# Causal convolution and token-mixing MLP on one core: x in 128-token chunks, convolution in 64x64 tiles, a VectorE block transpose, gated stores

## The reference, cut to what matters

```python
w = softmax(weight)                                   # 8 heads x 7 taps
y[b, s, h, g] = sum_k w[h, k] * x_pad[b, s + k, h, g] # 6 zeros ahead of each batch
W_tok = 1/8 * (y @ w_q) @ (y @ w_k).T                 # 4224 x 4224, a batch
out = relu(W_tok @ y) @ w_out                         # 4224 x 192, f32
```

## Time and profile before

| what | us |
|---|---|
| three runs | 170.98, 170.24, 170.30 |
| the profiled execution: its span, first to last instruction | 168.6 |
| median of the runs less that span: what lies around it | 1.7 |
| TensorE matmul busy | 158.3 (94% of the span) |
| TensorE weight loads busy (beside the matmuls) | 116.1 |
| ScalarE busy | 123.8 (73%) |
| VectorE busy | 116.2 (69%) |
| GpSimd busy | 30.3 |
| HBM read, written | 27.56 MB, 25.95 MB |

### The profile page before, as it was taken

How to read it: one execution, slowest core, us unless ns; L and a number is a source line. 1 busy time by engine, 2 the same in 40 slices (tenths; PEclk the granted TensorE clock), 3 DMA queues, 4 the chain that set the end, 5 groups by cost and what they waited for, 6 DMA issues and landing times.

```text
span 168.6 us, 6398 instructions
## 1 busy us (share of the span) xinstructions
PE 158.3 (94%) x2874; PEld 116.1 (69%) x2882; DVE 116.2 (69%) x201; ACT 123.8 (73%) x207; POOL 30.3 (18%) x39
## 2 busy tenths in 40 slices
PE   6978999999999999999999999999999999999980
PEld 1458846876677886777865867787778777884640
DVE  5745878774678777566999686875957758578640
ACT  3233699798977869888566978578897889568970
POOL 7999553530503120000000000000000000000000
PEclk9999999999999999999999999999999999999997
DMA  2999999999999999999999999996644463095897
GB/s 23 172 190 185 205 191 196 189 241 301 263 328 208 300 268 276 299 251 317 284 287 199 289 282 341 235 273 232 231 176 190 189 257 149 0 368 218 315 363 283
DMA packets 48154, 40.31 MB, mean 239 GB/s; under 512 B 37632, under 2 KB 40960, under 8 KB 48128
## 3 DMA queue, kind: packets, MB, share of 16 engines
q0 software_dynamic: 36128, 13.61, 67.6%
q1 hardware_dynamic: 12000, 26.31, 43.1%
HBM read 27.56 MB, written 25.95 MB: 317 GB/s over the span
## 4 chain that ended last, share of the span: by engine, by line
PE 78%; ACT 8%; DMA 4%; DVE 3%; issue 2%; POOL 1%; POOLq 0%; ACTq 0%
PE ps L744 14%; PE ps L902 12%; PE ps L920 9%; PE ps L316 8%; PE ps L321 5%; PE ps L836 5%; DMA out_dram<-out_sb 4%; PE ps L678 4%; PE ps L707 4%; ACT y L621 4%; PE ps L711 3%; PE ps L856 3%; PE ps L315 3%; PE ps L322 3%; PE ps L317 2%
## 5 line engine op out<-in xcount | busy, mean ns | idle before, releaser
L621 ACT CAST y<-ps 122x864 bf16<-122x864 f32 (+3 forms) x48 | 37.2, 794 | 11.6 <-PE ps L315 5.8
L873 ACT ACTIVATE rt<-ps 128x1024 bf16<-128x1024 f32 (+3 forms) x56 | 38.7, 725 | 8.3 <-PE ps L836 6.8
L941 ACT COPY out_sb<-ps 128x768 f32<-128x768 f32 (+1 forms) x43 | 32.6, 779 | 11.9 <-PE ps L920 11.3
L513 POOL DMA_DIRECT2D xw<-in_x_dram x34 | 29.9, 909 | 29.4 <-issue 28.6
L941 DVE COPY out_sb<-ps 128x768 f32<-128x768 f32 (+1 forms) x29 | 23.9, 831 | 14.0 <-PE ps L920 12.7
L744 PEld LDWEIGHTS ps<-y 122*64 122x64 bf16 x840 | 29.4, 110 | 5.3 <-issue 2.2
L744 PE MATMUL ps<-y 122*64 122x64 bf16 (+3 forms) x840 | 32.8, 221 | 0.1
L648 DVE COPY ytl<-ps 128x976 bf16<-128x976 bf16 (+1 forms) x40 | 23.3, 592 | 7.2 <-PE ps L321 4.1
L621 DVE CAST y<-ps 122x816 bf16<-122x816 f32 (+3 forms) x24 | 21.5, 902 | 8.1 <-PE ps L317 5.4
L316 PE MATMUL ps<-xw,band 128*64 128x408 bf16 (+2 forms) x104 | 24.9, 342 | 0.0
L317 PE MATMUL ps<-xw,band 128*64 128x408 bf16 (+2 forms) x104 | 24.9, 342 | 0.0
(11 more groups left out here) (117 smaller groups left out, 209.8 us busy)
## 6 DMA issues: line engine op xcount, KB each, us to landing
out_dram<-out_sb SPq DMA_DIRECT2D x28, 768.0 KB, 7.3
xw<-in_x_dram POOLq DMA_DIRECT2D x7, 816.0 KB, 40.3
xw<-in_x_dram POOLq DMA_DIRECT2D x7, 768.0 KB, 42.9
out_dram<-out_sb SPq DMA_DIRECT2D x8, 384.0 KB, 3.1
xw<-in_x_dram POOLq DMA_DIRECT2D x2, 432.0 KB, 7.3
out_dram<-out_sb SPq DMA_DIRECT2D x8, 96.0 KB, 5.1
xw<-in_x_dram POOLq DMA_DIRECT2D x1, 384.0 KB, 5.1
xw<-in_x_dram POOLq DMA_DIRECT2D x8, 45.8 KB, 28.0
```

The source lines that it names most:

```text
L513: lambda e, op, part=part: e.dma_start(*part),
L621: return e.copy(dst, src) if op.engine == "ACT" else e.tensor_copy(dst, src)
L873: return e.activation(dst, src(), AF.Relu)
L941: return e.copy(dst, src) if op.engine == "ACT" else e.tensor_copy(dst, src)
```

## The change

The whole program is declared and ordered anew; the arithmetic is the same.

- **Load.** A batch is 33 chunks of 128 tokens, each row read once, in 4 pieces (9, 8, 8, 8 chunks). `XW` is a ring of 3 batches with one zero chunk ahead, and a load waits until the convolution of three batches earlier has read its part.
- **Convolution.** 64x64 tiles: a chunk's lower and upper 64 rows are two row tiles, the 64 new outputs of each half two column tiles. A pair of heads takes two phases of four matmuls, one in each quadrant; the second (`conv_2`) adds into what the first wrote, and so waits for its end. The run-up of a chunk's first rows comes from the chunk before it. The evacuation is that of before, with 33 x 24 columns a head.
- **Transposes.** TensorE's are gone but for the last chunk (`gen_last`). VectorE turns `y` in 32x32 blocks of 4-byte words (pairs of channels), 4 instructions a batch (`gen_turn`), SBUF to SBUF.
- **Query.** One pass a batch: 48 matmuls of 32 rows x 64 columns, 512 columns each, into four banks; two evacuations of 1024 columns.
- **Output.** Units of 1024 tokens as before; the product with `w_out` has four forms, that `PLAN` picks (`x`, `y`, `z` or none). The last 128 tokens of a batch have a small path of their own (`l_...`).
- **Stores and order.** 12 output slots, 40 stores, all whole. An S entry of `PLAN` may name a load that must have landed first, as `274S373`. Weights are loaded at the start, and the weight casts and the set-up are spread over ScalarE and VectorE.

```diff
-NRT = 3
-NOUT = 4
-XW = sbuf("xw", [128, B, NCC, D], BF16)
+RING = 3
+NRT = 4
+NOUT = 12
+PIECES = [range(0, 9), range(9, 17), range(17, 25), range(25, 33)]
+XW = sbuf("xw", [128, RING, NC + 1, D])
...
+            if op.engine == "SP" and bank:
+                op.needs.append(self.ops[int(bank)])
...
     def gen_load(b, gi):
+        dst = XW[:, b % RING, 1 + c0 : 1 + c0 + n, :]
+        src = bass.AP(x_t, (b * S + 128 * c0) * D, [[D, 128], [128 * D, n], [1, D]])
+        load[b, gi] = add(
+            "load", "POOL", lambda e, op: e.dma_start(dst, src), n * 128 * D * 4,
+            needs=[op for c in range(c0, c0 + n) for op in conv_of.get((b - RING, c), [])],
...
     def gen_conv(b, gi):
+                o = [bank(op.bank + i)[:, 0 : n * GRP] for i in range(2)]
+                def one_(i, r, c, start, stop):
+                    h = 2 * hp + i
+                    rs, k = slice(64 * r, 64 * r + 64), 0 if (r, c) == (1, 0) else 1
+                    t = 64 if r != c else 0
+                    return (
+                        o[i][64 * c : 64 * c + 64], BAND[rs, h, t : t + 64],
+                        XW[rs, slot, c0 + k : c0 + k + n, GRP * h : GRP * h + GRP], start, stop, False,
+                    )
+                if not phase:
+                    yield one_(0, 0, 0, True, False)
+                    yield one_(0, 1, 1, True, False)
+                    yield one_(1, 0, 1, True, False)
+                    yield one_(1, 1, 0, True, False)
+                else:
+                    yield one_(0, 1, 0, False, True)
+                    yield one_(1, 0, 0, False, True)
+                    yield one_(0, 0, 1, False, True)
+                    yield one_(1, 1, 1, False, True)
...
+            mo = pe("conv_2", partial(conv, phase=1), holds=mm, vt=mm.vt + 0.01, info={"b": b}, vneeds={"": [(mm, True)]})
...
-    def gen_transpose(b, cs):
-    def gen_transpose_hi(b, g):
+    def gen_turn(b, cs):
+            lambda e, op: e.transpose(
+                T[:, yb, c0 : c0 + n, :].rearrange("p c d -> p (c d)").bitcast(U32),
+                Y[:, yb, c0 : c0 + n, :].rearrange("p c d -> p (c d)").bitcast(U32),
+            ),
...
     def gen_wq(b, turns):
+            for s in range(6):
+                j, e = divmod(s, 2)
+                for c in range(2):
+                    for g in range(4):
+                        p = slice(32 * g, 32 * g + 32)
+                        t = T[p, yb, HALF * c : HALF * c + HALF, :].rearrange("p c (j t e) -> p c j t e", j=3, e=2)
+                        yield bank(op.bank + g)[64 * c : 64 * c + 64, :], W32[p, j, e, :], t[:, :, j, :, e], s == 0, s == 5, False, (32 * g, 64 * c)
...
     def gen_unit(b, u, evm, evq):
+        def lo(op):
+            for r, c in ((0, 1), (1, 0), (0, 0), (1, 1)) if par else ((0, 0), (1, 1), (0, 1), (1, 0)):
+                yield bank(op.bank + r)[64 * c : 64 * c + 64, :], m_of(r, c), w_of(r), True, True, False
+        def hi(op):
+            for r in range(2):
+                c = r ^ par
+                yield bank(op.bank)[64 * c : 64 * c + 64, :], m_of(r, 2), w_of(r), True, True, False
...
+                if op.variant == "y":
+                    for q, lo, a in ((q, lo, a) for q in range(2) for lo in range(2) for a in range(2)):
+                        o, cols, p = bank(op.bank + a)[:, D * q : D * q + D], slice(2 * s + q, 512, 4), rows_of(a ^ par)
+                        yield o, RT[p, slot, a if lo else 2, cols], (WOL if lo else WOH)[p, :], q == 0 and not lo, False, False
...
+            fh = pe("f_hi", f_hi, needs=[rh, *casts_oh, *casts_oz], after=[fl], holds=fl, vt=vt + 0.07 + 0.01 * s,
+                vneeds={"y": [(fl, True)]}, info={"b": b, "variants": "xzy"})
```

More of the change, by code:

```diff
@@ L338, in emit, with copied, matmuls @@
+    def copied(dst, src):
+        return lambda e, op: e.copy(dst(op), src(op)) if op.engine == "ACT" else e.tensor_copy(dst(op), src(op))
+    def matmuls(make):
         def emit(e, op):
             last = None
-            for i in range(n):
-                if n == 6 and 1 <= i < 5:
-                    spare = (turned.bank + 3) % 7
-                    for r, c in ((0, 0), (1, 0), (0, 1), (1, 1)) if i < 3 else ((0, 0), (0, 1)) if i == 3 else ((0, 0), (1, 0)):
-                        p = slice(64 * r, 64 * r + 64)
-                        e.matmul(bank(GB if r else spare)[64 * c : 64 * c + 64, 0:512], RUNUP[p, 0:64], RUNUP[p, :], start=True, stop=True)
+            for o, l, r, start, stop, turn, *at in make(op):
+                if turn:
+                    last = e.transpose(o, l, r)
@@ L346, in emit @@
                 else:
-                    last = e.matmul(bank(GB)[:, 0:512], RUNUP[:, 0:128], RUNUP[:, :], start=True, stop=True)
+                    last = e.matmul(o, l, r, start=start, stop=stop, skip_group_check=True, tile_position=at[0] if at else None)
             return last
-        return add("PE", emit, 213.5 * n, needs=needs, after=after, mode=FULL, kind="run_up")
-    zero_r = add("DVE", lambda e, op: e.memset(RUNUP[:, :], 0.0), 200)
-    one = add("DVE", lambda e, op: e.memset(IDENT[:, :], 1.0), 100, vt=-9.5)
@@ L539, in bass_lightweight_conv__then__hypermixer_token_mlp_kernel, with spread, band, band_src @@
-    load_q = gen_weight("wq", wq_t, DH, QS, -3.0)
-    load_k = gen_weight("wk", wk_t, DH, KS, -2.9)
-    load_o = gen_weight("wo", wo_t, D, OS, -2.8)
-    def cast(dst, src, loaded, more=()):
-        return add("ACT", lambda e, op: e.copy(dst, src), 250, needs=[loaded, *more], vt=-4)
+        290, needs=[wn, own], vt=-9.23)
+    bands, fills = [], []
+    for half in range(2):
+        def spread(op, half=half):
+            for q in range(5):
+                o = 96 + KC - 1 - 16 * q
+                for c in range(2):
+                    yield (
+                        bank(op.bank)[64 * c : 64 * c + 64, 64 * q : 64 * q + 64].rearrange("p (i h) -> p i h", h=4),
+                        STEPT[0:112, o : o + 64],
+                        TAPS[0:112, :, 4 * half : 4 * half + 4],
+                        q == 0, q == 4, False,
+                    )
+        fill = pe("setup", spread, needs=[taps, stept], after=[warm_2, *fills], banks=1, vt=-9.2 + 0.01 * half)
+        fills.append(fill)
+        def band(op, half=half):
+            return BAND[:, 4 * half : 4 * half + 4, 0:80]
+        def band_src(op, fill=fill):
+            return bank(fill.bank)[:, 0:320].rearrange("p (t h) -> p h t", h=4)
+        bands.append(add("band", both, copied(band, band_src), 320, drains=fill, vt=-9.1))
@@ L546, in twice, with cast @@
+    warm_2_read = add(
+        "setup", "ACT", lambda e, op: e.copy(RUNUP[0:32, 0:2], bank(warm_2.bank)[0:32, 0:2]), 2, drains=warm_2, vt=-8.5)
+    def cast(dst, src, loaded, cols, more=(), vt=0.0):
+        return add("cast", ("ACT", "POOL", "DVE"), copied(lambda op: dst, lambda op: src), cols, needs=[loaded, *more], vt=vt,
+            info={"sbuf": True})
     def twice(ap):
         return ap.unsqueeze(1).to_broadcast([ap.shape[0], 2, DH])
+    casts_32 = [
+        cast(W32[32 * g : 32 * g + 32, :, :, :].rearrange("p j e n -> p j (e n)"), W32F[:, :, :], load_32, 384, vt=-3 + 0.1 * g)
+        for g in range(4)
+    ]
```

1087 lines of the change are left out of this document (443 added, 644 removed).

## The result

Four runs of the changed kernel took 157.31 to 158.75 us, median 158.3, against 170.3: a ratio of 0.9287, 95% interval 0.9249 to 0.9326. The forecast was 153.5 in a range of 144 to 168: faster as forecast, 4.8 us less so. The profiled execution took 157.31 us for a span of 155.2, so 2.1 us lie around it, where the sum had 1.7.

What follows compares the result with a forecast made beforehand. VectorE was to set the end, nearly level with TensorE: 9.9 start + 127 VectorE + 3 idle + 5 mutual waits + 3 end + 4 last store = 151.9 us span; with 1.7 around it 153.6, forecast 153.5, range 144 to 168.

Steps and rivals of the forecast that it cites:

- TensorE, 126 us: Sum of TensorE's matmuls, changes of shape and waits in the new kernel: 126 us, against 156 before.
- the prediction's 0.11: Price in us of one change of tile shape on TensorE; 116 changes were counted, 12.8 us.
- waits for itself: TensorE's second convolution phases and second output-product halves waiting for their first parts: 29 us if bare, taken as 7.
- the Gram price: TensorE's Gram product: 264 chunks at 0.082 us each, 21.6 us.
- VectorE, 127 us: VectorE's evacuations, casts and block turns: 128 us of work, 127 after the first convolution, taken to set the end.
- the 5 us that I gave to the two waiting for each other: Loss in the middle of the kernel, as TensorE and VectorE now and then wait for each other: 5 us.
- the estimate of 25.6 us: All VectorE block turns at the Trainium skill's rate of one element per cycle and lane; the forecast itself took 30.6 us.
- The start: ScalarE's early weight cast waits for its load, delaying the start by 1 us; first convolution evacuation at 9.9 us.
- DMA decides (0.17): Rival: transfers, with a floor of 143 us of span, stop the gain at 145 to 148 us; chance 0.17.
- Stores held too long (0.13): Rival: gated stores use up the 12 output slots and evacuations stop, 158 to 167 us; chance 0.13.
- Two row tiles in one bank take turns (0.07): Rival: convolution and third mixing product double on TensorE, 29 us more, 166 to 172 us; chance 0.07.
- The turn is dear (0.08): Rival: VectorE's turn of 768 words costs up to 1.74 us, 178.7 us; slower than before from 1.48; chance 0.08.

Runs made afterwards that it cites:

- without gates: Changed kernel with the loads that stores are held for taken out of the order list, so a store waits for its evacuations alone: 158.18 us.
- the shifted one: Against the kernel with thirteen run-up matmuls and four fillers, eleven run-up matmuls became 48 short ones, moving later TensorE instructions on by 37 places: 157.81 us.
- the three kernels with the cut second phase: Changed kernel, second convolution phase cut to one 24-column matmul: alone 155.21 us, with shorter convolution evacuations 154.52, with longer run-up and four added matmuls 154.89.
- the filled start: Changed kernel with thirteen run-up matmuls instead of nine and four more behind the first piece's convolution: 157.46 us; with the second phase cut too, 154.89.

## Why the prediction was right, and where it was wrong

- **TensorE, 126 us.** This step failed, by some 8 us: 133.8. Two of its prices held (quadrants in fours within 0.01 us and 0.18 to the next four where nothing is waited for; a query step 0.20 us for all eight 32x64 tiles). The failing term is what the convolution waits for itself: 22.4 priced, 32.3 measured, of which the 16 changes of shape behind it are some 1.8 at the prediction's 0.11. That leaves 8.1, and the output product, with 32 changes, has 3.7 left over in the same way, where the 7 us of "waits for itself" were to cover all of TensorE. A smaller miss is the Gram price: 0.082 us a chunk was read off one stretch, but a chain of 72 matmuls takes 2.22 us, 0.092 a chunk with the change of shape behind it and 0.089 within, and the kernel before has 0.089 on average: 1.8 us. The sentence that failed: "`PLAN` puts another operation between in most cases, so I take 7." In 45 of 72 pairs that is one other phase of the convolution, 0.19 us, in 8 it is nothing, and 0.43 are needed.
- **VectorE, 127 us, as the one that sets the end.** Its work was right (124.7), the turn to 1 ns. That it decides was wrong: 18 us less of it changed nothing. That 151.9 came out near 155.2 was luck: the two engines' sums were almost equal, and TensorE's own losses took the place of the 5 us that I gave to the two waiting for each other. (By the rate that the Trainium skill gives, "Vector Engine (DVE) Microarchitecture Reference", "The reshape front-end and per-opcode configuration", one element per cycle and lane, a word takes 1.04 ns at that page's 0.96 GHz; 1.02 were measured. What the estimate of 25.6 us left out is the fixed 0.17 us of each turn: 30.1 were measured.)
- **The start.** First convolution 8.42 for a forecast 8.9, the evacuation 9.14 for 9.9. The mechanism was right in kind, but at another place. The cast ahead of the exponential waited 1.92 us for its load, yet the exponential came at 4.54, where it had come at 4.51 before. A later cast, which waited 2.00 us, held the copy of `stept`. Moving that one changed nothing at the end.
- **DMA decides (0.17).** No: with 14 MB less the time fell by 3.7 us, not to another engine's floor. What the transfers cost shows, for 2.8 of the 3.0 us that this profile gained at its last matmuls, as stalls of TensorE at ends of instruction blocks.
- **Stores held too long (0.13).** No: without gates the time is the same, and no evacuation waits for a store.
- **Two row tiles in one bank take turns (0.07).** No: the four first-phase matmuls, of which two pairs write halves of one bank from different row tiles, start within 0.01 us, and the next four 0.18 later. (The Trainium skill, "TensorEngine Tiling (Array Packing)", "Gotcha 1: PSUM Pressure", has it that different row tiles cannot access one bank at the same time. By that the next four would come 0.36 us later, an estimate of two turns of 0.18; the measurement decides.)
- **The turn is dear (0.08).** No: 0.955 us, far from 1.48.

## What to carry to other kernels

Price a matmul that adds to what another has just written by the time from that one's start to its own (0.43 us here), and count what really stands between; its columns can be free. Where two engines' sums lie within some per cent, forecast from the one that has set the pace until now, and give its waits for itself more care than the other's work. Small tiles multiply instructions: at 128 matmuls a block of instructions, a stretch of short ones can outrun the reading of its own program, the more so while loads keep the transfers busy.

## What was not expected of the hardware

TensorE waited 0.76 to 1.16 us at ends of its instruction blocks in the changed kernel, and 1.65 in the shifted one. Each time it went on 1.2 to 1.6 us after a 16 KB read had ended. What stands at a block's end can be changed by adding matmuls far ahead.

The granted clock fell in five of the ten profiles of kernels with the whole convolution, for 3.4 or 6.8 us between 10.7 and 21.4 us. In the three kernels with the cut second phase it fell twice each, the second time at 89.6 us in two of them and at 25.0 in the third. From 10 to 17 us in the kernel after and in the one without gates:

```profile
10.00:17.00 7.00, 5.92 (x140) 3.49 (x140) 6.25 (x14) 3.50 (x10) 4.43 (x6) 1.00 1.60 192
```

```profile
10.00:17.00 7.00, 6.42 (x112) 4.44 (x112) 5.52 (x12) 2.73 (x7) 3.66 (x5) 0.57 1.60 192
```

The second was granted half its clock, 1.2 of 2.4 GHz, for most of these 7 us, after it had stood idle for 2.1 us ahead of the tap spread and 0.5 ahead of the second piece; the first had stood idle there for 1.5 and 0.6. It did 28 matmuls fewer, and its last matmul came 1.9 us later, of which 0.3 were lost before the clock fell. What decides whether it falls stays open: the filled start moved the fall from 10 us to 18 and did not end it.
